# Turning the block loop of a fused attention, MLP and mixture-of-experts kernel: the second relu half at the end of its own iteration, the change of expert spread over two iterations

## What is computed

```python
x = attention(q, k, v, 4 sinks, window 128)            # 4 batches, 8 heads, 768 positions, 64 wide
x = (h - tanh(h)) @ w_out   where h = x @ w_in         # 3072 tokens, 512 -> 2048 -> 512
e = argmax(x @ w_gate + modality_bias[modality_id])    # one of 8 experts for each token
p = softmax probability of that expert
out = p * (relu(x @ w1[e]) @ w2[e])                    # 512 -> 1024 -> 512, with the weights of expert e
```

## Time and profile before

| what | value |
|---|---|
| median of 3 runs | 1129.57 us (1126.35 to 1130.93) |
| the profiled execution: its own time | 1127.46 us |
| its span in the trace | 1125.9 us |
| TensorE busy (matmuls) | 1017.9 us, 90% of the span |
| VectorE, ScalarE, GpSimd busy | 729.1, 617.9, 399.3 us |
| chain that ended last, by engine | PE 63%, DVE 15%, issue 7%, ACT 7%, ACTq 3% |
| mean granted TensorE clock | 0.974 of full speed |

### The profile page before, as it was taken

How to read it: one execution, slowest core, us unless ns; L and a number is a source line. 1 busy time by engine, 2 the same in 40 slices (tenths; PEclk the granted TensorE clock), 3 DMA queues, 4 the chain that set the end, 5 groups by cost and what they waited for, 6 DMA issues and landing times.

```text
span 1125.9 us, 24616 instructions
## 1 busy us (share of the span) xinstructions
PE 1017.9 (90%) x7840; PEld 667.3 (59%) x7840; DVE 729.1 (65%) x2393; ACT 617.9 (55%) x1425; POOL 399.3 (35%) x457
## 2 busy tenths in 40 slices
PE   1667888999999999999999999999899899789996
PEld 0544555565666566566566566655577677567774
DVE  6787977677977867887877786647673334533231
ACT  2676877665776666667667576536412233422221
POOL 3786876322335322425422232011132222132221
PEclk9967999999999999999999999999999999899999
DMA  9832111241212331221141120041015111101111
GB/s 289 281 90 64 34 34 34 62 123 34 63 34 58 68 94 34 59 71 34 35 93 37 34 63 1 1 167 40 20 39 189 48 47 47 33 29 53 41 54 38
DMA packets 24427, 75.14 MB, mean 67 GB/s; under 512 B 9680, under 2 KB 9808, under 8 KB 22800
## 3 DMA queue, kind: packets, MB, share of 16 engines
q1 hardware_dynamic: 15440, 60.58, 19.9%
q0 software_dynamic: 5728, 13.43, 3.7%
q10 hardware_dynamic: 3168, 0.02, 0.1%
HBM read 60.16 MB, written 14.12 MB: 66 GB/s over the span
## 4 chain that ended last, share of the span: by engine, by line
PE 63%; DVE 15%; issue 7%; ACT 7%; ACTq 3%; POOL 2%; DMA 1%; DVEq 1%; SPq 0%; POOLq 0%
PE h_ps L710 16%; PE acc L766 15%; PE pt_ps L1799 9%; PE h_ps L1851 5%; PE x_out L669 4%; PE acc L1851 3%; PE s_ps L546 2%; ACTq L1631 2%; PE pt_ps L615 2%; DVE qk_exp L398 2%; DVE g_raw L731 2%; DVE qk_top L389 1%; PE s_ps L815 1%; ACT probs L561 1%; DVE g_lo L751 1%
## 5 line engine op out<-in xcount | busy, mean ns | idle before, releaser
L766 PE MATMUL acc<-w_out_all,g_hi 128*128 128x512 f16 x768 | 228.3, 379 | 0.0
L710 PE MATMUL h_ps<-xt_hi,w_in_all 128*128 128x384 f16 x960 | 197.3, 329 | 13.2 <-DVE g_raw L731 13.2
L766 PE MATMUL acc<-w_out_all,g_lo 128*128 128x512 f16 x384 | 145.5, 379 | 5.2 <-DVE g_lo L751 3.6
L598 ACT ACTIVATE pt_hi<-pt_ps 128x256 f16<-128x256 f32 (+2 forms) x224 | 83.6, 380 | 109.4 <-PE pt_ps L615 104.8
L710 PEld LDWEIGHTS h_ps<-xt_hi,w_in_all 128*128 128x128 f16 x960 | 91.7, 98 | 67.6 <-issue 10.3
L99 POOL TENSOR_TENSOR tick<-tick 1x1 f32<-1x1 f32 x83 | 16.3, 196 | 291.0 <-ACT y L1867 132.1
L1816 DVE SCALAR_TENSOR_TENSOR hid_lo<-pt_ps,hid_hi 128x512 f16<-128x512 f32 x50 | 34.5, 691 | 130.3 <-ACT hid_hi L1813 124.9
L751 DVE SCALAR_TENSOR_TENSOR g_lo<-g_raw,batch_scale,g_hi 128x384 f16<-128x384 f32 x128 | 95.2, 744 | 33.1 <-ACT g_hi L741 30.7
L766 PEld LDWEIGHTS acc<-w_out_all,g_hi 128*128 128x128 f16 x768 | 75.0, 98 | 69.0
L602 DVE TENSOR_TENSOR pt_lo<-pt_ps,pt_hi 128x256 f16<-128x256 f32 (+2 forms) x224 | 94.3, 423 | 28.9 <-ACT pt_hi L598 27.4
L436 POOL TENSOR_TENSOR q_stack<-qk_raw,q_stack 64x768 f16<-64x768 f32 x31 | 50.8, 1640 | 165.5 <-ACT q_stack L432 165.5
(11 more groups left out here) (300 smaller groups left out, 2282.9 us busy)
## 6 DMA issues: line engine op xcount, KB each, us to landing
qk_raw<-in_qk SPq DMA_DIRECT2D x64, 454.0 KB, 6.0
raw<-in_w SPq DMA_DIRECT2D x16, 512.0 KB, 8.7
v_raw<-in_v SPq DMA_DIRECT2D x4, 1536.0 KB, 9.5
x_tokens<-x SPq DMA_DIRECT2D x24, 256.0 KB, 5.0
w_in_all<-in_w_in SPq DMA_DIRECT2D x4, 1024.0 KB, 12.9
w_out_all<-in_w_out SPq DMA_DIRECT2D x4, 1024.0 KB, 12.1
x_tokens<-g_raw SPq DMA_DIRECT2D x1, 1024.0 KB, 13.8
slots<-payload,dest POOLq DMA_INDIRECT x24
```

The source lines that it names most:

```text
L598: eng.activation(pt_hi[:, at, :], out, ACT.Copy).then_inc(q["pt_hi_done"], 1)
L710: mm = eng.matmul(h_of(m, f), w16[0][:, f, x * DM + k * P:x * DM + (k + 1) * P], r[:, par, k, :], start=(i == 0), stop=(i == 3 * KD - 1))
L766: mm = eng.matmul(acc[t][:, :], l[f % 2][:, t * P:(t + 1) * P], w16[1][:, f, x * DM:(x + 1) * DM], start=(f == 0 and i == 0), stop=(f == N ...
```

## The change

One code word, `event`, says what is due: 0 nothing, 3 the look (iteration F-3), 1 scales and both halves of w1 (F-1), 2 both halves of w2 (F). TensorE's, GpSimd's and SyncE's programs are the same, apart from the semaphore that starts the late loads. The core of the diff:

```diff
-        if E in ("act", "dve"):
-            begun, earlier = read(eng, 4, j, NE), read(eng, 4, j - 1, NE)
-            looking, following = read(eng, 2, j - 1, NE), read(eng, 4, j + 1, NE)
-            value = read(eng, 0, j - 1, NE * N - P) if E == "act" else turn_of(eng, j - 1)
-            next_turn_ends(E, eng, j, begun, earlier)
-            relu(E, eng, j - 1, 1)
-            output_part(E, eng, j - 1, 1 - p, value)
+        if E == "act":
+            event, s = read(eng, 2, j, 3), read(eng, 3, j, NE, lo=1)
+            before_half(E, eng, j, event, s)
             scale_x(E, eng, j + 1, 1 - p)
-            next_scales(E, eng, following)
             relu(E, eng, j, 0)
-            next_turn_begins(E, eng, j, following, begun)
+            load_slots_again(E, eng, j - 1)
+            after_half(E, eng, j, event, s)
             transpose_x(E, eng, j + 1, 1 - p)
-        if E == "act":
-            load_slots_again(E, eng, j - 1, value)
-            look_ahead(E, eng, looking)
+            at_end(E, eng, j, event, s)
+            relu(E, eng, j, 1)
             output(E, eng, j - 1, 1 - p)
         if E == "dve":
+            event, s, turn = read(eng, 2, j, 3), read(eng, 3, j, NE, lo=1), turn_of(eng, j)
+            scale_x(E, eng, j + 1, 1 - p)
+            before_half(E, eng, j, event, s)
+            relu(E, eng, j, 0)
+            after_half(E, eng, j, event, s)
+            transpose_x(E, eng, j + 1, 1 - p)
             output_scale(E, eng, j - 1, j - EARLY)
-            look_ahead(E, eng, looking)
+            at_end(E, eng, j, event, s)
+            relu(E, eng, j, 1)
+            output_part(E, eng, j, p, turn)
+            finish_look(E, eng, j, event, s)
```

More of the change, by code:

```diff
@@ new lines, in plan_late @@
+        event, turn, look, begun = metaf[:, 2, :], metaf[:, 3, :], vec["e"], metaf[:, 4, :]
+        w, m = MB - 4, MB - 1
+        step(ts(b[:], now, 1.0, None, ALU.add))
+        step(ts(t[:], b[:], mv["turn_end"][:, TURNS - 1:TURNS], None, ALU.is_lt))
+        step(tt(b[:], b[:], t[:], ALU.mult))
+        step(tt(sel[:, 0:w], now[:, 0:w], now[:, 3:w + 3], ALU.is_equal))
+        step(tt(sel[:, 0:w], sel[:, 0:w], first[:, 4:MB], ALU.mult))
+        step(tt(t[:, 0:w], first[:, 0:w], first[:, 3:w + 3], ALU.mult))
@@ new lines, in plan_late @@
+        step(tt(sel[:, 0:w], sel[:, 0:w], t[:, 0:w], ALU.add))
+        step(tt(look[:, 0:w], sel[:, 0:w], b[:, 0:w], ALU.mult))
+        step(tt(begun, first[:], now, ALU.mult))
+        step(ts(turn, begun, 1.0, None, ALU.max))
+        step(tt(turn[:, 0:m], turn[:, 0:m], begun[:, 1:MB], ALU.max))
+        step(tt(turn[:, 1:w + 1], turn[:, 1:w + 1], look[:, 0:w], ALU.max))
+        step(ts(sel[:], begun, 0.0, None, ALU.is_gt))
+        step(ts(t[:, 0:w], look[:, 0:w], 0.0, None, ALU.is_gt))
+        step(ts(event, sel[:], 2.0, None, ALU.mult))
@@ L1637, in load_turn @@
     def load_turn(eng, s):
-        e = read(eng, 3, s, NE - 1)
+        e = read_turns(eng, s, NE - 1)
         for i in range(PIECES):
@@ L1817, in relu, with load_slots_again @@
                .then_inc(q["hid_lo"], 1)
-    def load_slots_again(E, eng, j, row=None):
+    def load_slots_again(E, eng, j):
         if E == "act":
-            if row is None:
-                row = read(eng, 0, j, NE * N - P)
+            row = read(eng, 0, j, NE * N - P)
             need(eng, q["scattered"], 16 * j)
@@ L1971, in last_output @@
         if E == "act":
-            relu(E, eng, last, 1)
             load_slots_again(E, eng, last)
@@ L1975, in last_output @@
         if E == "dve":
-            relu(E, eng, last, 1)
-            output_part(E, eng, last, last % 2, turn_of(eng, last))
             output_scale(E, eng, last, regular + 1)
```

112 lines of the change are left out of this document (68 added, 44 removed).

## The result

| | before | changed kernel |
|---|---|---|
| median (range, runs) | 1128.24 us (1126.35 to 1130.93, 4) | 1110.8 us (1109.66 to 1114.72, 4) |
| the profiled execution: its time, its span | 1127.46, 1125.9 us | 1110.36, 1108.4 us |
| TensorE busy | 1017.9 us, 90% | 1011.9 us, 91% |
| transposes of block 5 to those of block 25 | 243.8 us | 224.8 us |
| start of the last 24 matmuls to their end | 5.37 us | 6.96 us |

The ratio is **0.985**, interval 0.982 to 0.988: faster by 1.5%. The forecast was 1109.1 with a range of 1103.5 to 1115. The loop gave 19.0 us; 1.6 were lost behind it.

A forecast was written before the change was run, and what follows sets the result against it. TensorE was held to wait for the previous block's relu half 1, losing 24.2 us in the loop. 24.2 - 0.5 - 3.2 = 20.5 us less than 1127.46 gives 1107.0; adding 2.1 for the median, 1109.1 us, range 1103.5 to 1115.

The forecast's parts named there:

- the prediction's signs: Across the loop: transposes 10.98 us apart nearly everywhere, full clock, waits only in iterations 5 and 11 and behind 13.
- The first pass: Loop's first two steps, from block 5's transposes: 5.4 us lost before, 0.5 us to stay, through `scale_x` of block 6.
- that move: Issuing the `slot_y` DMA ahead of ScalarE's transposes: costs nothing, as long as the scatter has landed.
- The undisturbed steps: The other 14 loop steps: all 2.9 us lost there go, since relu half 1 is ready at T+1.4, needed at T+5.4.
- Reads: worth nothing by itself: Reads per iteration, five to three on ScalarE and VectorE: no gain, as TensorE waits for neither after the change.
- VectorE's reads run beside the waiting `hid_lo`: VectorE at the iteration's start: its sequencer fetches on past the waiting instruction, so 2.2 us are not paid.
- The rival: VectorE's reads are held behind the waiting relu: 2.2 us more, 1111.3 us; chance 0.12.
- The change of expert: Four steps around the expert switch: of 15.9 us lost, 3.2 stay (1.3 in iteration 11, 1.9 in 13); bounds 0 to 8.
- just in time: Iteration 12, ahead of the expert switch: `scale_x` done near T+3.7, `xg_lo` ready at T+10.9, no loss.
- The end: Behind the loop: nothing lost, since `y` of the last but one block, 0.65 us later, fits TensorE's 2.40 us late start.
- The bound of 0 to 0.65: Limits in us on the loss at joining and behind the loop, from `y` coming 0.65 later; 0 was taken.

The follow-up runs named there:

- the kernel with the half put back: Changed kernel with relu half 1 moved back behind the reads of the following iteration (two on ScalarE, three on VectorE): 1106.49 us, ratio 0.981.
- the turn alone: Kernel before with only relu half 1, and the splits that must stand ahead of it, moved to its own iteration's end: 1123.56 us, ratio 0.996.
- Experiment 5: Changed kernel with ScalarE's issue of the `slot_y` read moved back behind its transposes of x: 1109.79 us, one run.
- five reads and two dead branches at the head: Changed kernel with relu half 1 back in the next iteration, behind five reads on each engine and two more never-taken branches: 1117.81 us, one run.
- reads doubled: Changed kernel with VectorE's three reads at the iteration's start done twice, the first results unused: 1132.38 us, one run.
- the late spread: Changed kernel with SyncE's second DMA of the statistics held until block 12's output scale has been taken: 1107.63 us.

## Why the prediction was right, and where it was not

The total was right: 18.8 us less than the median shown before were measured where 20.5 were forecast, and in the same runs 17.4. The pace, the clock at full speed in the loop, and the waits of iteration 11 and behind 13 came as the prediction's signs had them; the wait of 2.21 us behind iteration 12 was not among them. That the total came out does not vouch for its reasons: by the same reasons the kernel with the half put back had to take 1116 to 1118 us, and it took 1106.5.

1. **The first pass: right, and better.** 0.5 us were to stay, none did. `slot_y` was there 1.4 us earlier than I took it (`y_scale` at 869.12, not 870.5), and the reads behind `hid_lo`, dearer than the 2.1 us I gave them (2.5 from its end, 3.2 from its start), took part of that back: `scale_x` was done at 874.8 where 875.6 was forecast. Experiment 5 shows that the earlier issue of `slot_y` matters here: without it 1.8 are lost, in one run. I had priced that move at nothing everywhere.
2. **The undisturbed steps: right in size, wrong in cause.** The 2.9 us went. But the turn alone leaves them at 11.03 and 11.25, and without the turn they are at 10.98 too, even with five reads and two dead branches at the head. So it was not the earlier half. What it was stays open: the look in one piece, and the last 0.4 to 0.8 us of the old head, were not put back.
3. **"Reads: worth nothing by itself" was the step that failed.** Three more on ScalarE and two on VectorE cost 6.2 to 7.1 us in the loop when the half stands at the head, and three on VectorE alone cost 19.6 in the changed kernel (24.8 against 5.2), an estimate of 3.4 of them by half clock.
4. **"VectorE's reads run beside the waiting `hid_lo`" failed with it.** They begin with `hid_lo`. The rival had this at 2.2 us; taking them out of the way gave 1.9 to 2.5 (4.6 or 5.2 less 2.7). So that rival is true, and the 1110.8 measured lies nearer to its 1111.3 than to the forecast's 1109.1. The gain itself was missed by 3.1 us: 0.5 better in the first pass, 2.0 worse at the change and 1.6 worse at the end. That the total lies only 1.7 off is luck in part, as the median before came out 1.3 lower than the one that the forecast started from. The Trainium skill (Perfetto Trace Analysis, "DVE / Act Engine Instruction") has a waiting instruction go to a wait queue and the sequencer fetch on. For these register reads the trace does not agree: of the 4.82 us above none fell into the 1.86 us of waiting ahead of them. Whether the sequencer stands still or the read itself waits for what is queued was not taken apart.
5. **The change of expert: 3.2 forecast, 5.2 measured.** Iteration 11's wait of the transposes for the scaled tokens was forecast at 1.3 and took 1.04 and 0.30. Iteration 13 was forecast at 1.9 and took 1.39 (the step behind it). Iteration 12, "just in time", took 2.44 (2.00 in the second profile): held reads, of which moving them away shows little here since the splits then start no earlier (12.98 stays), 0.95 from the group of the outer loop that begins there, which I had not looked for (0.5 of it would come back in the next step), and 0.4 that one of two executions lost, the one with the slower `slot_y`.
6. **The end: 0 forecast, 1.6 measured**, all half clock. The bound of 0 to 0.65 was made from who waits, and had no term for the clock.

The loop gave 19.0 for 20.5 and the end took 1.6, and the profiled span fell by 17.5. As to where the 19.0 came from: with half 1 put back and a head of five reads and two dead branches 13.9 of 24.2 are gone already, which the look in pieces, the order of splits and `slot_y`'s place share, together with the half clock that no longer follows (an estimate of 5.9 us before); their shares were not taken apart. Fewer reads bring 6 to 7; the turn itself is worth 4.6 us to the old loop and costs 0.5 to 1.1 in the new one.

## What to carry to other kernels

In this kernel a register read on an engine that computes cost 0.5 to 0.7 us and began only with the last instruction ahead of it, so its place counts like that of a compute instruction: put it behind what others wait for, and pack conditions into fewer words. Where a change has several parts, the one that names it need not be the one that pays; undo each alone, as the part that pays may be worth more without it. And a loop in longer groups can pay behind the loop for iterations that it skips: here 1.4 us of idle time, and 1.2 to 2.8 in TensorE's clock.

## What the runs showed of the hardware that was not expected

The half clock. Behind the loop the idle time was 2.36 to 2.40 us in eleven executions; the last 24 matmuls took 5.36 to 5.37 us in seven of them, at full clock, and 6.96 to 7.05 in four (the changed kernel twice, `slot_y` put back, and the head with two branches). An idle time of 3.75 to 3.80 us was followed by half clock in three of three, and 1.82 and 2.21 in the loop were not. But in the loop too it went either way: an idle time of 2.08 us was followed by half clock with five reads and with the reads doubled, and twice not with five reads and two branches; 2.05 (reads doubled) was followed by it, 2.16 (half turned alone) was not. The two executions below have the same program behind the loop and the same idle time, and the chain that ended last shows one of each kind, the changed kernel and then the one with the late spread:

```profile
1094.86 6.96 PE h_ps L1841 x24
```

```profile
1093.74 5.37 PE h_ps L1843 x24
```

What decides between them isn't in these rows. At idle times like these a forecast has to carry both, 1.6 us apart.

Two branches that are not taken moved nothing that could be read (3.01 against 3.03 us), while three reads beside them moved 1.6.
